# Rows of x for the expert stage: turned by a transposing transfer instead of by TensorE

## What is computed

```python
N, D, E, F = (1792, 768, 8, 1024)
...
e_idx = np.argmax(logits, axis=1)
...
for e in range(E):
    mask = e_idx == e
    h = np.maximum(x[mask] @ w1[e], 0.0)
    ye = h @ w2[e]
    out[mask] = gate_w[mask, None] * eom[mask, e, None] * ye
```

## Time and profile before

| | |
|---|---|
| median of 3 runs | 1086.53 us (1086.39 to 1090.44) |
| profiled execution, its own time | 1086.73 us |
| its span, first to last instruction | 1085.0 us |
| TensorE busy over the span | 1065.9 us, 98% |
| VectorE, ScalarE, GpSimd busy | 577.7, 428.5, 241.8 us |
| mean granted TensorE clock | 0.998 of full speed |
| start of tile 0 and end of the last matmul | 766.1 and 1077.2 us |

### The profile page before, as it was taken

How to read it: one execution, slowest core, us unless ns; L and a number is a source line. 1 busy time by engine, 2 the same in 40 slices (tenths; PEclk the granted TensorE clock), 3 DMA queues, 4 the chain that set the end, 5 groups by cost and what they waited for, 6 DMA issues and landing times.

```text
span 1085.0 us, 17675 instructions
## 1 busy us (share of the span) xinstructions
PE 1065.9 (98%) x6464; PEld 555.3 (51%) x6465; DVE 577.7 (53%) x867; ACT 428.5 (39%) x613; POOL 241.8 (22%) x211
## 2 busy tenths in 40 slices
PE   7999999999999999999999999999999999999996
PEld 3444434444555555555555555556555555555554
DVE  7799999983433333333332320015583754655741
ACT  5788888885211111111111210001451542543431
POOL 4687877831000000000000100000112121121111
PEclk9999999999999999999999999999999999999999
DMA  6267877541412111111100541010673654555710
GB/s 156 60 140 137 171 158 158 119 94 36 140 60 59 58 59 53 56 49 56 47 1 1 164 142 44 29 43 16 246 254 103 249 176 145 187 187 196 272 35 19
DMA packets 117593, 118.61 MB, mean 109 GB/s; under 512 B 71600, under 2 KB 93486, under 8 KB 117536
## 3 DMA queue, kind: packets, MB, share of 16 engines
q1 hardware_dynamic: 113952, 106.37, 33.8%
q0 software_dynamic: 3168, 11.02, 3.0%
q10 hardware_dynamic: 416, 0.47, 0.1%
HBM read 99.49 MB, written 13.85 MB: 104 GB/s over the span
## 4 chain that ended last, share of the span: by engine, by line
PE 84%; issue 7%; POOL 6%; DMA 1%; DVE 0%; ACT 0%; SPq 0%; POOLq 0%; DVEq 0%; ACTq 0%
PE ps L1689 30%; PE ps L1704 15%; PE ps L1783 12%; PE ps L1761 12%; PE ps L1585 5%; POOL arena L664 3%; PE ps L1559 3%; PE ps L1770 1%; POOL arena L650 1%; PE ps L1748 1%; POOL arena L654 1%; PE ps L1536 1%; POOL arena L671 1%; PE ps L1576 1%; PE ps L1830 1%
## 5 line engine op out<-in xcount | busy, mean ns | idle before, releaser
L1689 PE MATMUL ps<-arena 128*128 128x448 f16 x1728 | 328.8, 352 | 0.0
L1689 PEld LDWEIGHTS ps<-arena 128*128 128x128 f16 x1728 | 168.2, 98 | 156.1 <-issue 0.5
L1704 PE MATMUL ps<-arena 128*128 128x392 f16 (+1 forms) x996 | 165.3, 329 | 0.0
L1250 DVE SCALAR_TENSOR_TENSOR arena<-arena 128x768 f16<-128x768 f32 (+1 forms) x112 | 113.2, 1066 | 66.2 <-ACT arena L965 65.3
L1761 PE MATMUL ps<-arena 128*128 128x512 f16 x648 | 145.6, 379 | 0.8 <-DVE arena L1449 0.8
L1783 PE MATMUL ps<-arena 128*128 128x384 f16 x816 | 135.4, 326 | 0.0
L1704 PEld LDWEIGHTS ps<-arena 128*128 (+1 forms) x996 | 97.3, 98 | 66.9
L932 ACT ACTIVATE arena<-ps 128x448 f32<-128x448 f32 x48 | 26.1, 543 | 258.0 <-PE ps L1689 258.0
L1585 PE MATMUL ps<-arena 128*128 128x448 f32 x288 | 126.6, 562 | 0.0
L1224 DVE SCALAR_TENSOR_TENSOR arena<-ps,arena 128x448 f32<-128x448 f32 x48 | 30.0, 624 | 171.7 <-PE ps L1689 92.8
L965 ACT ACTIVATE arena<-arena 128x768 f16<-128x768 f32 (+1 forms) x112 | 99.7, 928 | 44.0 <-DMA arena<-in_moe_w 40.3
(11 more groups left out here) (186 smaller groups left out, 993.3 us busy)
## 6 DMA issues: line engine op xcount, KB each, us to landing
arena<-in_moe_w SPq DMA_DIRECT2D x48, 512.0 KB, 5.5
arena<-in_moe_w SPq DMA_DIRECT2D x64, 384.0 KB, 4.8
arena<-in_qk SPq DMA_DIRECT2D x23, 448.0 KB, 4.7
y_parts<-arena SPq DMA_DIRECT2D x16, 384.0 KB, 2.3
arena<-sums_inv SPq DMA_DIRECT2D x48, 112.0 KB, 2.9
arena<-in_v SPq DMA_DIRECT2D x24, 192.0 KB, 2.9
arena<-in_moe_w_gate SPq DMA_DIRECT2D x12, 384.0 KB, 4.2
arena<-in_moe_w_val SPq DMA_DIRECT2D x12, 384.0 KB, 5.7
```

The lines of the kernel that those rows point to most:

```text
L1250: nc.vector.scalar_tensor_tensor(lo, raw_rows(e, p), S_OP, hi, ALU.mult, ALU.subtract).then_inc(w_lo_ready, 1)
L1689: last = nc.tensor.matmul(ps[:, 2 * (b % 2) + g, 0:S], up_w[s][:, g, c, wl], xt[:, b * KC + c, xl], start=(c == 0 and wl + xl == 0), stop= ...
L1704: last = nc.tensor.matmul(ps[:, 4 + 2 * s + h, 0:cols], gt[:, f, gl, bass.ds(t * 128, 128)], wo[:, f, wl, h, 0:cols], start=(f == 0 and gl ...
```

## The change

The twelve transposes of `turn_rows` are taken off TensorE for the tiles 2 and later. Instead ACT issues one transposing DMA for each tile (`move_rows`), which turns the 128 x 1536 f16 of `x_rows` in 12 blocks into a new SBUF buffer `x_next`. In the list of ACT for tile g the issue for tile g + 1 stands right behind `hidden` of half 0. It waits for the gathered rows and for the copy of the tile before out of `x_next`. DVE's `rows_out` waits for both halves of `up` of tile g (they read `x_t`) and for the transfer, and makes one copy of 128 x 1536 f16 from `x_next` to `x_t`. The gather of tile g + 2 waits for the transfer of tile g + 1 instead of for the transposes. Tiles 0 and 1 keep the old way.

```diff
--- before.py
+++ after.py
@@ -236,6 +236,7 @@
             homes = w2_home if x == 0 else []
             w2_s.append([a.rearrange("p (l f) -> p l f", l=2) for a in
                          homes + [m2.take(128, 2 * DM, F16) for _ in range(F2C - len(homes))]])
+        x_next = m2.take(128, 2 * DM, F16)
         hid = m2.take(128, F2, F32)
         hid_parts = m2.take(128, 2 * F2, F16).rearrange("p (l f) -> p l f", l=2)
         hid_t = m2.take(128, 2 * F2, F16).rearrange("p (b l c m) -> p b l c m", b=2, l=2, c=4)
@@ -364,6 +365,7 @@
         second_sent = sem("second_sent")
         gathered = sem("gathered")
         rows_turned = sem("rows_turned")
+        rows_moved = sem("rows_moved")
         x_t_ready = sem("x_t_ready")
         hid_sum = sem("hid_sum")
         hid_ready = sem("hid_ready")
@@ -704,7 +706,7 @@
             def gather(g):
 
                 if not isinstance(g, int):
-                    read, turned, copied = pool.to_reg(16 * g), pool.to_reg(2 * g), pool.to_reg(g + 1)
+                    read, turned, copied = pool.to_reg(16 * g), pool.to_reg(16 * g - 32), pool.to_reg(g + 1)
                     pool.wait_ge(route, ROUTE_DONE)
                     pool.wait_ge(gathered, read)
                 else:
@@ -719,7 +721,7 @@
                 else:
                     pool.wait_ge(y_stored[1], 8 * TT)
                     pool.wait_ge(gather_idx_ready, copied)
-                    pool.wait_ge(rows_turned, turned)
+                    pool.wait_ge(rows_moved, turned)
                 nc.gpsimd.indirect_dma_start(out=x_rows, out_offset=None, in_=y_dram,
                                              in_offset=bass.IndirectOffsetOnAxis(ap=gather_idx, axis=0),
                                              bounds_check=last_row, oob_is_err=False).then_inc(gathered, 16)
@@ -781,6 +783,7 @@
                                              bounds_check=last_half_row, oob_is_err=False).then_inc(scattered, 16)
             pool.wait_ge(scattered, 16 * last + 48)
             pool.wait_ge(gathered, 16 * last + 48)
+            pool.wait_ge(rows_moved, 16 * last)
 
         @block.scalar
         def _(act):
@@ -1002,11 +1005,21 @@
                 nc.scalar.activation(hid[:, b * 512:(b + 1) * 512], ps[:, b, :], ACT.Relu, scale=1.0 / S_OP)\
                     .then_inc(hid_ready, 1)
 
+            def move_rows(g):
+
+                landed, free = act.to_reg(16 * g + 16), act.to_reg(g)
+                act.wait_ge(route, ROUTE_DONE)
+                act.wait_ge(gathered, landed)
+                act.wait_ge(x_t_ready, free)
+                act.dma_start_transpose(x_next.rearrange("p (b m) -> p b m", m=128), x_rows).then_inc(rows_moved, 16)
+
             def tile(e, s, before, first):
                 g = before + 1
                 if first:
                     split_high(e, s, range(KC + 5, PIECES) if is_at(g, 0) else range(KC, KC + 4))
                 hidden(g, 0)
+                if not is_at(g, 0):
+                    move_rows(g + 1)
                 if first and not is_at(g, 0):
                     split_high(e, s, range(KC + 4, PIECES))
                 hidden(g, 1)
@@ -1443,6 +1456,10 @@
             def rows_out(g):
 
                 wait(dve, hid_sum, 2 * g)
+                if not (is_at(g, 0) or is_at(g, 1)):
+                    dve.wait_ge(rows_moved, 16 * g - 16)
+                    nc.vector.tensor_copy(x_t.rearrange("p l c m -> p (l c m)"), x_next).then_inc(x_t_ready, 1)
+                    return
                 bank = 2 if is_at(g, 0) else 6
                 for l in range(2):
                     dve.wait_ge(rows_turned, 2 * g + l + 1)
@@ -1794,7 +1811,8 @@
                     turn_hidden(before, 0)
                     turn_hidden(before, 1)
                 up(e, s, g, 1, first)
-                turn_rows(g + 1)
+                if is_at(g, 0):
+                    turn_rows(1)
                 pe.wait_ge(hid_ready, 2 * g + 1)
                 if not is_at(g, 0):
                     if first:
```

## The result

| | before | after |
|---|---|---|
| median (range) of 5 runs each | 1086.98 us (1086.39 to 1090.44) | 1104.61 us (1100.01 to 1121.81) |
| ratio after to before | | 1.0139, 95% interval 1.0123 to 1.0155 |
| a second set, 6 runs (`after_again`) | 1086.57 us | 1108.32 us (1091.75 to 1115.92), ratio 1.0121 (1.0063 to 1.0178) |
| span of the profiled execution | 1085.0 us | 1102.7 us (of `after_again`) |

The change makes the kernel slower by 1.4%, some 15 us, where the forecast had 10.5 us less. The ratios leave out executions more than 1.5% above the fastest of their kernel (two of the 5, three of the 6), the medians do not, and the rows of after are those of an execution of the second set that counts (1104.41 us). The quotients of the medians are 1.016 and 1.020, so 1.2 to 1.4% is the lower side of the loss.

What follows compares the result with a forecast made beforehand. TensorE's chain was taken to bound the kernel; 1086.73 us less 10.9 us for 17 transpose groups gave 1075.8, rounded to 1076.0 us for small waits. Clean range 1074.6 to 1079 us; 8-in-10 range 1074.6 to 1098 us.

Steps and rivals of the forecast that it cites:

- What bounds the kernel: Expert stage: the chain from tile 1 on is TensorE alone, 17.13 us a tile; what leaves its list leaves the time.
- The term of 10.9 us: Gain from 17 transpose groups leaving TensorE: 16 x 0.67 = 10.7 us, plus 0.2 us in tile 1.
- The transfer alone: The new transposing transfer lands 4.0 us after issue when the DMA engines are free; bounds 3.2 and 7.4 us.
- The issue on ACT: Issuing the 12-block transfer takes ACT 1.3 to 2.2 us, taken as 2.0, covered by about 4 us.
- The rival in which the issue holds ACT for over 4 us in first tiles: `rows_down` of the tile behind waits 1 to 2 us in six tiles, about 1083 us; counted within partly starved, 0.18.
- The copy on DVE: DVE's copy of 1536 f16 from `x_next` takes 0.42 to 1.25 us, taken as 0.8, ending before x_t is needed.
- Company on the DMA engines: In six first tiles weights keep the engines busy during the transfer; forecast landing after about 5 to 6 us.
- the starved case: Rival: in first tiles small packets wait one by one for weight packets; landing 12.7 us, total 1094 us; chance 0.30.
- the queueing term: Starved rival's wait in first tiles: 54 weight packets per engine at 0.162 us ahead of the transfer's packets.
- the 18 us of the rival: Starved rival's loss: about 3 us in each of six first tiles, 1075.8 + 18 = 1094 us; chance 0.30.
- The rule weighed against the trace: Skill's packets of 9 to 17 descriptors give landings of 5 to 6 us; the trace's start shows single rows alternating.
- The signs named beforehand: Wrong if TensorE idles before `up` behind DVE's copy or `rows_down` behind `turned_hidden`; only first tiles: company; all: the transfer.

Runs made afterwards that it cites:

- paced: Changed kernel, transfer issued at the head of ACT's tile, SP holding each expert's pieces from the eighth until the previous expert's second-tile transfer lands; 1077.78 us, ratio 0.9922.
- half_rows: Changed kernel with ACT's transfer turning only the high parts, 768 packets in place of 1536; 1076.88 us, ratio 0.9913.
- light_after: Changed kernel with only 16 columns of the weights loaded for experts 2 to 7, packets of 64 B; 1077.6 us, ratio 0.9903.
- plain_copy: Changed kernel with an ordinary copy of the same bytes, 128 rows of 3 KB, in place of the transposing transfer; 1077.19 us, ratio 0.9908.
- small_copy: Changed kernel with a copy in 1536 packets of 248 B, nothing turned, in place of the transposing transfer; 1082.09 us, ratio 0.9937.

## Why the prediction was wrong

**What bounds the kernel: right.** The chain was TensorE's list alone, and what left it left the time wherever nothing new came late. `paced` (but for three tiles), `half_rows`, `light_after` and `plain_copy` have tiles of 16.46 us from tile 2 on and end at 1076.9 to 1077.8 us, 9.2 to 10.5 us below the kernel before beside them. The term of 10.9 us holds to within 0.4 to 1.7 us.

**The transfer alone: right.** Predicted 4.0 us, bounds 3.2 to 7.4; 3.7 to 5.7 in `light_after`, 4.1 at best in after. The Trainium skill (VectorE: DVE Perf Modes, "The three transpose paths") has 1309 ns for one block of 128 x 128 by DMA; these rows show twelve blocks in one transfer landing within 3.7 us, about 0.3 us a block with all fixed costs, so the measurement disagrees with a reading of that figure as a price for each block of many.

**The issue on ACT: partly right.** Predicted 1.3 to 2.2 us, taken at 2.0; the median is 2.02 and the maximum 3.0. In `light_after` the median is 1.47 and the maximum 2.5, so the larger part of the issues is longer beside the weights, but some are above 2.2 us without them. The rival in which the issue holds ACT for over 4 us in first tiles did not decide anything: 3.0 us is the longest here, and in the other profiled execution of after (1121.81 us) one issue took 4.6 us, in a second tile.

**The copy on DVE: right within the bounds,** 0.56 us (predicted 0.42 to 1.25, taken at 0.8). It was near the quick end.

**Company on the DMA engines: the step that failed.** The forecast took a landing of 4 to 6 us for the first tiles as likeliest, though the earlier trace rows had shown single packets of both queues taking turns, and gave the starved case 0.30. It was the starved case: in six tiles the transfer took 13.0 to 19.0 us, against a room of some 10 us. Three terms of that case were also too small:

- *The landing.* 12.7 us were worked out at 0.021 us for a small packet and 0.162 us for one of the weights. A transfer with that many packets but without turning landed after 13.5 us in tile 2 and after 6.3 to 14.9 us in the five other loaded first tiles, so the queueing term was right in size for the worst tiles. The turning one took 19.0 us in tile 2, where both kinds of packet are slower: 0.045 and 0.234 us. Nothing in the trace of before had a transposing transfer in company, and the bounds from rows of one alone did not hold for it.
- *Where.* I had six first tiles. Tiles 2, 3 and 12 to 15 are the ones in the trace of after, so three of the six are second tiles. The earlier trace rows already had the company there: its stretch with a DMA share of 0.93, which the prediction counted to the first tile, is 862.30 to 870.00, the first 7.7 us of tile 6, a second tile. The text had the scatter, its index and `rows_done` coming late behind a late transfer, but did not follow this into the next tile: the weights come late, ACT's splits and `rows_done` with them, the next transfer is issued late (821.39, 5.8 us into tile 3) among the loads of the next expert, and lands after 13.02 us. Tiles 13 and 15 are alike (issued 6.8 and 6.6 us into the tile). On the other side tiles 5, 7 and 10 were clean in this execution: their transfers landed after 8.9, 6.8 and 6.7 us, and in the second tiles behind them they were issued 4.3 to 4.6 us into the tile and landed in time (9.7, 11.3 and 6.0 us). The time of after differs by up to 24 us from one execution to the next, and what decides how many tiles are hit stays open.
- *The clock.* It was not in the sum at all. Behind a gap of 7.23 us TensorE has the granted clock of 0.50 for 3 us. Over the stage this is 9.1 of the 30.7 us, some 30%.

With the idle time of 20.3 us alone, close to the 18 us of the rival, the sum would have been 1075.8 + 20.3 = 1096 us, within the range. The 9.1 us of the clock take it out, to 1105 us.

**The rule weighed against the trace: the trace was right.** The Trainium skill (DMA: Bandwidth & Descriptors, "Queues, rings and completion order") has an engine go round its queues by packets that are typically 9 to 17 descriptors. By that the transfer would have landed after 5 to 6 us. `small_copy` took 13.5 us in tile 2, where 1148 packets of the weights went beside its 1552, and `plain_copy`, with nearly the same bytes in a twelfth of the rows, at most 6.6 in all tiles; no such grouping shows here. The quickest loaded tile of `small_copy` (6.3 us, tile 10) would fit the rule as well.

**The signs named beforehand** were the right ones: idle time ahead of the first matmul of `up`, released by the copy. But they stand behind first and second tiles, and not behind all.

## What to carry to other kernels

A transfer that takes an engine's work off the path is only as good as its landing in the worst company it meets: count its packets (here 96 per engine), ask what else is in the queues then, and let the nearest row in company, not the one alone, carry the forecast. If it must be small packets, issue it ahead of the bulk loads and hold these back until it has landed: that turned +1.4% into -0.8% here, while either half of it alone left the kernel slower than before. Where a gap of some microseconds opens in TensorE's work, look at the granted clock behind it and price that too.

## What was not expected of the hardware

- A transposing transfer beside loads of the weights can slow everything on the DMA engines: 208 GB/s against 362 with the same number of copied small packets, 512 KB landing after 16.0 us against 6.7, and 19.0 us against 13.5 for itself. So it was in tile 2; in tiles 7 and 10 of the same execution the transfer landed after 6.8 and 6.7 us, at 0.018 and 0.020 us a packet. The cause inside the DMA engines is open.
- Small packets in one queue wait among large ones of another, and their number bears on the landing: 4.4 to 5.3 us in the loaded first tiles of `plain_copy` with 128 rows, 6.3 to 14.9 us in those of `small_copy` with 1536.
- The granted clock was 1.00 up to a gap of 7.3 us, 0.75 as a mean in it, 0.50 in the 3 us behind it and 0.97 after that; over the stage the lower level cost 9.1 us in five places. Behind the shortest of the six gaps (1.29 us) no matmul was slow.
- A copy of 128 x 1536 f16 in SBUF takes VectorE 0.56 us, 2.7 numbers per ns and partition; the cast of 512 numbers took 0.416 us, which is 1.2.
